# Attention and two mixtures of experts: weights as the stationary operand, in high and low parts, in passes of up to 416 tokens

## What is computed

```python
x = attention(q, k, v)             # 4 sink keys and a window of 128, then (1536, 512)
# first mixture: each expert takes 192 tokens, by greedy capacity routing on x @ w_gate
for e in range(8):
    h = np.maximum(x[assigned == e] @ w1[e], 0.0)       # 192 x 512 @ 512 x 1024
    out[assigned == e] = h @ w2[e]                      # 192 x 1024 @ 1024 x 512
x = out
# second mixture: two experts for each token, by noisy logits
noisy = x @ w_gate2 + np.log1p(np.exp(x @ w_noise)) * noise
top2 = argpartition(-noisy, 2)[:, :2];  top2_w = softmax of the two
for e in range(8):
    for k in range(2):
        mask = top2[:, k] == e
        out[mask] += top2_w[mask, k, None] * (np.maximum(x[mask] @ m2_w1[e], 0.0) @ m2_w2[e])
```

## Time and profile before

| | us |
|---|---|
| median of 3 runs (lowest, highest) | 911.54 (909.22, 921.75) |
| the profiled execution | 913.54 |
| its span | 911.94 |
| attention and first logits | 0 to 150 |
| capacity routing, then scatter | 150 to 319.8 |
| first mixture | 319.8 to 515 |
| second routing | 515 to 555.3 |
| second mixture | 555.3 to 896.4 |
| tail | 896.4 to 911.9 |

### The profile page before, as it was taken

The page is one execution under the profiler, slowest core; times in us unless marked ns, Lnnn a source line. Parts: engine busy times, 40 slices in busy tenths (PEclk is TensorE's granted clock), DMA queues, the critical chain, the costliest instruction groups (busy, mean ns, idle before and its releaser), DMA issues.

```text
span 911.9 us, 16773 instructions
## 1 busy us (share of the span) xinstructions
PE 751.2 (82%) x5353; PEld 661.4 (73%) x5354; DVE 381.5 (42%) x913; ACT 280.4 (31%) x536; POOL 99.1 (11%) x114
## 2 busy tenths in 40 slices
PE   3999996444444099999999667999999999999993
PEld 2898995334443099999999565887788788888882
DVE  5444443999988000000000382644444462536221
ACT  2455653000000022332222302443344452535210
POOL 2000000000000500000000001222122212122220
PEclk9999997555555589999999857999999999999997
DMA  9700002900000446666660301645264453454211
GB/s 219 206 2 1 1 2 70 407 35 0 0 0 0 163 138 212 230 228 224 244 231 27 110 0 36 214 128 149 57 202 136 138 160 93 127 138 120 53 27 30
DMA packets 63908, 103.91 MB, mean 114 GB/s; under 512 B 22336, under 2 KB 24384, under 8 KB 63872
## 3 DMA queue, kind: packets, MB, share of 16 engines
q1 hardware_dynamic: 54896, 80.05, 26.9%
q0 software_dynamic: 8976, 23.39, 10.0%
HBM read 87.64 MB, written 16.57 MB: 114 GB/s over the span
## 4 chain that ended last, share of the span: by engine, by line
PE 73%; issue 18%; DMA 3%; DVE 2%; POOL 1%; ACT 0%; SPq 0%; DVEq 0%; POOLq 0%; ACTq 0%
PE PS L737 12%; PE PS L739 11%; PE PS L738 11%; PE PS L670 9%; PE PS L659 8%; PE PS L502 4%; PE PS L465 3%; PE PS L482 3%; PE PS L733 3%; DMA XE<-routed_rows 2%; PE PS L717 2%; PE PS L726 1%; PE PS L443 1%; POOL routed_rows L391 1%; PE PS L680 1%
## 5 line engine op out<-in xcount | busy, mean ns | idle before, releaser
L1141 DVE TENSOR_TENSOR WS<-STAGE,WS 128x1024 f32 (+1 forms) x64 | 74.7, 1221 | 232.6 <-ACT WS L872 197.1
L737 PE MATMUL PS<-WS,XH 128*128 128x512 f32 x216 | 89.7, 415 | 3.9 <-DVE XL L1257 2.0
L620 PE MATMUL PS<-OH,arena 128*128 128x8 bf16 x1008 | 39.8, 169 | 61.2 <-DVE arena L1119 59.2
L659 PE MATMUL PS<-XTm,arena 128*128 128x192 f32 x512 | 88.4, 333 | 1.1 <-ACT XTm L855 1.1
L737 PE MATMUL PS<-WS,HH 128*128 128x512 f32 x216 | 88.8, 411 | 0.0
L659 PEld LDWEIGHTS PS<-XTm,arena 128*128 128x128 f32 x512 | 85.8, 195 | 1.3 <-issue 1.3
L739 PE MATMUL PS<-WS,XL 128*128 128x512 f32 x216 | 85.4, 395 | 0.0
L670 PE MATMUL PS<-HTm,arena 128*128 128x192 f32 x512 | 84.8, 327 | 0.5 <-ACT HTm L861 0.5
L738 PE MATMUL PS<-WS,XH 128*128 128x512 f32 x216 | 85.0, 394 | 0.0
L739 PE MATMUL PS<-WS,HL 128*128 128x512 f32 x216 | 84.6, 392 | 0.0
L738 PE MATMUL PS<-WS,HH 128*128 128x512 f32 x216 | 84.4, 391 | 0.0
(11 more groups left out here) (227 smaller groups left out, 1140.7 us busy)
## 6 DMA issues: line engine op xcount, KB each, us to landing
arena<-in_moe_w SPq DMA_DIRECT2D x16, 2048.0 KB, 8.9
STAGE<-in_moe_w SPq DMA_DIRECT2D x128, 256.0 KB, 4.8
XE<-routed_rows SPq DMA_DIRECT2D x8, 390.8 KB, 9.8
arena<-in_v SPq DMA_DIRECT2D x12, 256.0 KB, 6.4
out<-YO POOLq DMA_DIRECT2D x1, 3072.0 KB, 20.3
first_mixture<-YR POOLq DMA_DIRECT2D x16, 192.0 KB, 4.4
arena<-in_q SPq DMA_DIRECT2D x2, 1024.0 KB, 7.7
arena<-in_k SPq DMA_DIRECT2D x2, 1024.0 KB, 8.5
```

The costliest lines, as they stand in the source:

```text
L620: ins = pe.matmul(PS[:, 6, u * E:(u + 1) * E], CMP[:, t, u * P:(u + 1) * P], OH[:, t, :], start=False, stop=(t == NT - 1 and u == NT - 1), ...
L659: ins = pe.matmul(PS[:, 2 + f % 2, 0:CAP], W1[:, pp, c, f * P:(f + 1) * P], XTm[:, c, :], start=(c == 0), stop=(c == KD - 1))
L737: pe.matmul(acc, high, w_high, start=first, stop=False)
L1141: dve.tensor_tensor(part(1), STAGE[:, slot].rearrange("p o w f -> p (o w) f"), part(0).bitcast(F32), ALU.subtract)\
```

## The change

- The first mixture takes the form of the second one's products: weights and tokens split in high and low fp32r parts, three matmuls a product.
- In both mixtures the weights are the stationary operand (`product` now gets them first); the tokens are the moving one, 192 columns in the first mixture and always 416 in the second. The hidden values come out turned already, so the turned blocks of line 733 go; results are turned back at the end of a pass.
- The weights of an expert lie as 8 units of 512 KB (unit j < 4 holds two hidden blocks of w1, unit 4 + d one output block of w2), rearranged so on the host. There is one ring `WS` of eight units, high and low, and eight staging buffers. When a unit has been used, ScalarE and VectorE convert the next expert's into its place (`convert`), in program order with their other work, and SP loads the one after that into staging. Only units 0 to 3 of the first expert are loaded during capacity routing; 4 to 7 follow the scatter.
- A hidden block goes from PSUM bank 2 + f % 2 by ScalarE (relu, rounded) to `HH` and by VectorE (`hidden_low`) to `HL`; the block after next waits for that low part.
- The rows of the first mixture are written to `first_mixture` in token order by an indirect DMA, so the table needs two values instead of three.
- The second mixture has passes of up to 416 assignments of one expert, each with four groups of rows (128, 128, 128, 32): four gathers, four results, four scatters. Routing counts passes instead of tiles; there can be up to 15.

ScalarE, first mixture:

```diff
+            def convert(j, turn):
+                act.wait_ge(sm[STAGES[j]], turn)
+                act.activation(WS[:, 0, j, :], staged(j), ACT.Copy).then_inc(sm["whigh"], 1)
+            def expert(e, last):
+                for f in range(KF):
+                    act.wait_ge(sm["h1_ps"], e * KF + f + 1)
+                    act.activation(HH[:, f, 0:CAP], bank(2 + f % 2, CAP), ACT.Relu).then_inc(sm["h1high"], 1)
+                    if f % 2:
+                        convert(f // 2, e * 16 + 32)
                 for d in range(KD):
-                    act.wait_ge(sm["y_ps"], e * KD + d + 1)
...
+                    act.wait_ge(sm["y1_ps"], e * KD + d + 1)
+                    act.activation(YT[:, d, 0:CAP], bank(4 + d % 2, CAP), ACT.Copy).then_inc(sm["y1_out"], 1)
+                    if d == 2 and not last:
+                        rows_high(0, e * 2 + 3)
+                    if d == 3 and not last:
+                        rows_high(1, e * 2 + 4)
+                    convert(4 + d, e * 16 + 32)
...
+            for j in range(4):
+                convert(j, 16)
+            rows_high(0, 1)
+            rows_high(1, 2)
+            for j in range(4, 8):
+                convert(j, 16)
+            with act.Fori(0, E - 1) as e:
+                expert(e, False)
```

TensorE, the product and an expert of the first mixture:

```diff
-                pe.matmul(acc, high, w_high, start=first, stop=False)
...
+            def product(acc, w_high, w_low, high, low, first, last):
+                pe.matmul(acc, w_high, high, start=first, stop=False)
+                pe.matmul(acc, w_high, low, start=False, stop=False)
+                return pe.matmul(acc, w_low, high, start=False, stop=last)
...
+            def expert(e, last):
+                pe.wait_ge(sm["x1low"], e * 2 + 2)
+                for f in range(KF):
+                    if f % 2 == 0:
+                        pe.wait_ge(sm["wlow"], e * 8 + f // 2 + 1)
+                    if f == 1:
+                        pe.wait_ge(sm["l2_out"], AHEAD["l2_out"] + e)
                     if f >= 2:
...
+                        pe.wait_ge(sm["h1low"], e * KF + f - 1)
+                    hidden(f, CAP).then_inc(sm["h1_ps"], 1)
                 for d in range(KD):
+                    pe.wait_ge(sm["wlow"], e * 8 + 4 + d + 1)
                     if d >= 2:
...
+                        pe.wait_ge(sm["y1_out"], e * KD + d - 1)
                     for f in range(KF):
+                        if d == 0 and f >= KF - 2:
+                            pe.wait_ge(sm["h1low"], e * KF + f + 1)
+                        ins = outputs(d, f, CAP)
+                    ins.then_inc(sm["y1_ps"], 1)
+                    if d == 1 and not last:
+                        pe.wait_ge(sm["xe"], e * 16 + 32)
+                        turn_rows(0)
+                if not last:
+                    turn_rows(1)
+                pe.wait_ge(sm["y1_out"], e * KD + KD)
```

TensorE, a pass of the second mixture:

```diff
+            def one_pass(t, ex):
+                pe.wait_ge(sm["x2low"], t * KD + KD)
...
+                    hidden(f, NP).then_inc(sm["h2_ps"], 1)
+                pe.wait_ge(sm["yo"], t * NG + AHEAD["yo"])
...
+                    if d == 1:
+                        pe.wait_ge(sm["gath"], t * 16 * NG + 2 * 16 * NG)
+                        turn_gathered(0)
+                    if d == 2:
+                        turn_gathered(1)
+                for k in range(2, KD):
+                    pe.wait_ge(sm["x2low"], t * KD + KD + k - 1)
+                    turn_gathered(k)
+                pe.wait_ge(sm["y2_out"], t * KD + KD)
+                for g in range(NG):
+                    rows = rows_of(g)
+                    for d in range(KD):
+                        ins = pe.transpose(PS[0:rows, R_BANKS[g], d * P:(d + 1) * P], YT[:, d, g * P:g * P + rows], ident[:])
+                    ins.then_inc(sm["r2_ps"], 1)
```

VectorE:

```diff
+            def convert(j, count):
+                dve.wait_ge(sm["whigh"], count)
+                dve.sem_inc(sm["dve_held"], 1)
+                dve.tensor_tensor(WS[:, 1, j, :], staged(j), WS[:, 0, j, :].bitcast(F32), ALU.subtract).then_inc(sm["wlow"], 1)
+
+            def hidden_low(f, n, high, count, low):
+                dve.wait_ge(high, count)
+                dve.sem_inc(sm["dve_held"], 1)
+                dve.scalar_tensor_tensor(out=HL[:, f, 0:n], in0=bank(2 + f % 2, n), scalar=0.0, in1=HH[:, f, 0:n].bitcast(F32),
+                                         op0=ALU.max, op1=ALU.subtract).then_inc(low, 1)
...
+                for f in range(KF):
+                    hidden_low(f, CAP, sm["h1high"], e * KF + f + 1, sm["h1low"])
+                    if f % 2:
+                        convert(f // 2, e * 8 + 8 + f // 2 + 1)
...
+                for a in range(2):
+                    dve.wait_ge(sm["r1_ps"], e * 2 + a + 1)
...
+                    dve.tensor_copy(YO[0:HC, a, :], bank(6 + a, DM, HC)).then_inc(sm["r1_out"], 1)
```

SP, the first weights:

```diff
+            for j in range(4):
+                load_unit(m1_w1, m1_w2, 0, j)
             sp.wait_ge(sm["scat"], 16 * NT)
-            load_rows(0, 0)
+            load_rows(0)
             sp.dma_start(NZ[:], xs[:, DM:XC].rearrange("(g p) e -> p g e", p=HC)).then_inc(sm["nz_in"], 16)
...
+            for j in range(4, 8):
+                load_unit(m1_w1, m1_w2, 0, j)
```

More of the change, by code:

```diff
@@ L19, in build @@
     DV = D + 2
-    E, _, F = m1_w1.shape
+    E = m1_w1.shape[0]
+    F = m1_w1.shape[1] * 2 * P
     QT = S // P
@@ L729, in turn_hidden @@
-            def turn_hidden(t, c2):
-                pe.wait_ge(sm["hrelu"], t * 2 + c2 + 1)
-                for i in range(4):
-                    f = c2 * 4 + i
-                    ins = pe.transpose(PS[:, 3 + c2, i * P:(i + 1) * P], HB[:, f * P:(f + 1) * P], ident[:])
-                ins.then_inc(sm["ht_ps"], 1)
-            def product(acc, high, low, w_high, w_low, first, last):
-                pe.matmul(acc, high, w_high, start=first, stop=False)
-                pe.matmul(acc, high, w_low, start=False, stop=False)
-                return pe.matmul(acc, low, w_high, start=False, stop=last)
```

674 lines of the change are left out of this document (312 added, 362 removed).

## The result

The changed kernel takes 951.0 us (median of four runs, 946.3 to 956.5), the kernel before 912.5: a ratio of 1.0405, 95% interval 1.0342 to 1.0468, so slower. The profiled execution has a span of 945.0 us against 911.9, 33.1 us more.

What follows compares the result with a forecast made beforehand. TensorE's issue was taken to bound both mixtures. Terms 11.5 + 5.2 - 0.7 + 9.9 - 9.9 + 4.7 = +20.7 us took the profiled 913.54 to 934.2, 932 us against the median; range 899 to 960.

Steps and rivals of the forecast that it cites:

- rival B: First mixture: the chain of high part, low part and converts binds each pair, four 0.8 us stalls an expert, 951 us; chance 0.16.
- A product of 192 columns, 110 ns by the load: First mixture's products: the weight load sets the pace, 192 x 0.110 = 21.12 us, +0.29 us an expert.
- Rivals A: Products cost their stream, not their load: 192 columns about 90 ns, 416 about 184; 899 to 905 us; chance 0.22.
- C: Load and stream disturb each other: 17 ns on top of the load, 127 ns a product, 958 us; chance 0.12.
- One stall of 0.8 us an expert, bounds none and four: First mixture's hidden blocks: TensorE waits once an expert for a bank's low part, 0.8 us of a 25.13 us period.
- Start of the first mixture, +5.2, less 0.7: First expert: late units, a 2.8 us wait, second cold start, low part of rows, +5.2 us; last expert's row wait goes, -0.7.
- Between the mixtures, +9.9: Routing stretch between the mixtures: more operations, wider table steps, four gathers awaited, longer turning of rows; +9.9 us, bounds 5 and 14.
- Second mixture, -9.9: Second mixture: eight passes of 41.4 us, 331.2 against 341.1 us for 27 tiles, -9.9 us; bounds -28 and -7.
- Tail, +4.7: End of the kernel: four scatters in a row end 8.95 us after TensorE instead of 4.24, +4.7 us.

Runs made afterwards that it cites:

- the grouped kernel: Changed kernel with the two cross products in bf16, each block issuing its high x high fp32r products first, then its cross products: 918.1 us, 1.0036 of before.
- the second start: Changed kernel with the first expert's eight units loaded and ScalarE's parts made ahead of the scatters, VectorE's low parts held until the scatters landed: 954.4 us.
- the spread turns: Changed kernel with the next pass's four turned blocks behind output blocks 0, 1, 2 and 3 instead of 1, 2, 3 and 3: 939.05 us.
- the first version of the start: Changed kernel with units 4 to 7 of the first expert also loaded and converted ahead of the rows, VectorE's part as early as possible: 952.5 us.

## Why the prediction was right, and where not

The forecast was 932 us and slower; measured were 951.0, inside the range of 899 to 960 but outside the 920 to 945 that the prediction gave to its own mechanism. It is the very number of rival B, by chance: B's four stalls did not come. By steps, on the profiled execution:

- *A product of 192 columns, 110 ns by the load.* Right: 111, and with it the reason why three products gain nothing on two records. The runs with 208, 256 and 320 columns show the load as the pace up to about 250 columns. Rivals A (90 ns) and C (127 ns) both fall. The 17 ns that C wanted to add belong to the long stream (0.189 us against 0.173 for 416 columns, 16 ns) and not to the load.
- *One stall of 0.8 us an expert, bounds none and four.* It was one, of 0.6, and the period 25.26 instead of 25.13; the difference is in the products, 0.1117 us on average. Rival B (four stalls) falls. Four banks take the stall away: 0.6 us an expert here, 1.2 on the grouped kernel.
- *Start of the first mixture, +5.2, less 0.7.* Right in sum, with other parts. To the end of its products the mixture lost 17.7 us; eight periods of +1.57 are 12.6 of it, and 5.1 are left, where 4.5 were forecast. The wait before block 2 was 3.19 (2.8 forecast). It ended with VectorE's low part, behind the four conversions of the late units, and ScalarE's conversions ahead of these waited for each unit to land (0.2 to 0.4 us each from 323.8 on, 1.2 in all). The slow scatters were not foreseen: the rows are turned 22.3 us behind the first scatter instead of 21.1, +1.2. From the turned rows to the first product it is 2.87 us instead of the 2.57 of before, +0.3 (0.7 forecast). The second cold stretch came; no row had given the 1.7 us that the prediction put on it, and at half pace its 6.1 us cost 3.0. In both stretches TensorE worked at the lower level for 9.7 us, where the kernel before has 5.3 (322.40 to 327.72); 4.4 us more at half pace are 2.2. These make 6.9, which is 1.8 more than is left. Of that, 0.9 is what the kernel before lost in its last full period (24.59 instead of 23.69, with the wait of 0.7) and the changed one does not, and 0.6 is the stall, which the first expert, late already, does not have. The last 0.3 was not traced.
- *Between the mixtures, +9.9.* Right, also in its parts: from the last product to the first gather 37.9 us instead of 35.4 (+2.5, forecast 2.75), a step of the table 1.85 us on VectorE as forecast, and from the first gather to the first product 13.2 instead of 6.5 (+6.7, forecast 7.1).
- *Second mixture, -9.9.* This is the step that failed: +1.8. The product was right (188 ns forecast, 189 measured), and nearly so the wait (1.45; 1.25). The price of the turned blocks was what failed: "32 turned blocks x 0.11 = 3.5" carried the 0.11 of groups of four 128-row blocks over to groups whose fourth block has 32 rows. There the trace shows weight loads that no longer run ahead, and 0.70 us a group instead of 0.44. The two groups between products cost 1.4 us instead of 0.9. From the last product of a pass to the next pass it is 4.9 us instead of the forecast 4.4 (8 + 16 blocks, wait, seam), though the wait was 0.2 shorter. With 0.2 from the products that is 1.2 us a pass, 9.6 in eight. That the 32 rows are the cause is read from the trace; no run has groups without them. The cold start of the first pass, 2.2 us, had no term at all.
- *Tail, +4.7.* Right: +4.4.

The forecast for the profiled execution was 934.2 us, and it took 946.7, 12.5 more: 11.7 in the second mixture, 1.7 in the first, less about 1 in the other two terms. The rest of the distance from 932 to 951 lies between that execution and the medians: it lay 4.3 under the median of its four, and that of before 2.0 over the median that the forecast started from.

The change did what it says. It was slower because its new form pays a weight load for every 192 columns, which turns 128 records of 0.163 us into 192 products of 0.111 and gains nothing, while the chain of high and low parts, the start, the routing and the tail each got longer. The products of the second mixture saved 8 us (27 x 48 of 0.230 against 8 x 192 of 0.189), and the eight waits of 1.25 us alone took 10.

## What to carry to other kernels

Before splitting an fp32 product in three, compare its columns with its load: here a load of 128 columns set the pace up to some 250 moving columns, so three products of 192 cost what one fp32 product had, and only wider passes or a form that loads faster could win. If bf16 will do for the small products, group them by form within a block, and give the hidden blocks of such a chain four banks. Carry the price of a group of turned blocks over only to groups of the same shape: one block of 32 rows among blocks of 128 made a group cost 0.70 us instead of 0.44. And when two kernels are compared by single traces, begin the comparison behind the stretch that varies of itself, here attention.

## What the runs showed of the hardware that was not expected

- With 96 columns a product, TensorE's clock stayed at its lower level over whole experts (0.50 in a period in which the engine was busy for all of its 46.30 us), where with 192, 256 and 320 columns it stood at 1.00. Half the columns made the expert 1.8 times as long. The upper level came back at 746.0 us, 4.0 behind the first product of 208 columns.
- The upper level came 3.5 to 6.0 us behind the first product of the first mixture in eleven traces, and 12.6 and 13.5 us behind it in two (the second start, the spread turns), one of which has the changed kernel's own code up to there. What decides it stays open.
- At the lower level products of 96, 192 and 208 columns all start 0.213 us apart, twice the 0.111 of 192 columns at the upper one.
- A block of 32 rows, turned between blocks of 128, starts 0.202 us behind the one before instead of 0.109: its weight load is not issued ahead, and neither is that of the product behind it. Groups of 96-row blocks do not show this (starts 0.08 us apart, the load of the product behind them issued ahead, 348.58 to 348.86).
- Indirect DMAs took 1.84 to 1.97 us on POOL instead of 0.96 while VectorE converted weights.
- Alternating fp32r and bf16 products of 192 columns cost 0.303 us for one and two, the same products grouped by form 0.284.

Attention has two speeds, with the same code, and they are the clock's. The chain of waits has the same eight matmuls of attention in the changed kernel and in the first version of the start:

```profile
39.72 0.84 PE PS L483 x8
```

```profile
39.82 1.60 PE PS L481 x8
```
